# A mixture-of-experts layer: the second expert's weights are chosen and loaded before the last tokens are routed

## The reference, cut to what matters

```
logits = x @ w_gate                       # (2304, 8)
e_idx  = argmax(logits, axis=1)
gate_w = softmax(logits)[e_idx]
eom    = 1 / (1 + exp(-(x @ w_output_gate)))
for e in range(8):
    mask = e_idx == e
    if not mask.any(): continue
    h  = maximum(x[mask] @ w1[e], 0)      # 512 -> 1024
    ye = h @ w2[e]                        # 1024 -> 512
    out[mask] = gate_w[mask] * eom[mask, e] * ye
```

## Time and profile before

| | us |
|---|---|
| median of 3 runs (907.34 to 909.07) | 908.56 |
| the profiled execution | 907.39 |
| its span, first to last instruction | 905.5 |
| PE busy | 874.1 (97%) |
| DVE busy | 395.5 (44%) |
| ACT busy | 268.3 (30%) |
| POOL busy | 163.6 (18%) |
| DMA traffic | 68.50 MB, mean 76 GB/s |

### The profile page before, as it was taken

One profiled execution on the slowest core, in us unless ns is written; L12 is line 12 of the kernel. 1 busy time (PEld: TensorE's weight loads), 2 busy tenths in 40 slices (PEclk: granted clock), 3 DMA queues, 4 the chain that ended last, 5 costly groups with the idle time before them and its releaser, 6 DMA issues.

```text
span 905.5 us, 21892 instructions
## 1 busy us (share of the span) xinstructions
PE 874.1 (97%) x8248; PEld 784.0 (87%) x8249; DVE 395.5 (44%) x872; ACT 268.3 (30%) x499; POOL 163.6 (18%) x226
## 2 busy tenths in 40 slices
PE   8999999999999999999999999999979999999994
PEld 6888898989999898999989999898758888888883
DVE  5777885324233242333424233245754233624431
ACT  4564453222222122222212122226233113423311
POOL 5875301600000000000000000000123322323321
PEclk9999999999999999999999999999999999999997
DMA  9885733301010100001000010005161115216100
GB/s 264 245 233 165 234 113 114 95 12 36 4 44 0 39 8 12 35 0 46 0 23 23 12 35 0 24 1 210 34 224 47 35 46 183 85 38 213 52 25 19
DMA packets 52898, 68.50 MB, mean 76 GB/s; under 512 B 11886, under 2 KB 37614, under 8 KB 52848
## 3 DMA queue, kind: packets, MB, share of 16 engines
q1 hardware_dynamic: 46000, 45.20, 15.6%
q0 software_dynamic: 6560, 22.56, 8.1%
q10 hardware_dynamic: 288, 0.02, 0.0%
HBM read 54.11 MB, written 14.70 MB: 76 GB/s over the span
## 4 chain that ended last, share of the span: by engine, by line
PE 90%; DMA 3%; issue 2%; DVE 2%; SPq 1%; ACT 0%; POOLq 0%; POOL 0%; ACTq 0%; DVEq 0%
PE bank L1213 35%; PE bank L1234 15%; PE bank L1328 11%; PE bank L1356 11%; PE bank L1105 4%; PE bank L1182 4%; PE bank L1129 4%; PE bank L1343 2%; DMA e_w<-w 2%; PE bank L1165 1%; PE bank L1279 1%; PE bank L1243 1%; PE bank L1203 1%; DMA k_sb<-kT 1%; PE bank L1252 1%
## 5 line engine op out<-in xcount | busy, mean ns | idle before, releaser
L888 DVE TENSOR_TENSOR prod<-silu,bank 128x256 f32<-128x256 f32 x108 | 45.5, 421 | 209.5 <-ACT silu L597 209.2
L1213 PE MATMUL bank<-x_hi,wg_hi 128*128 128x256 f32 x432 | 125.2, 290 | 0.0
L1213 PE MATMUL bank<-x_hi,wv_hi 128*128 128x256 f32 x432 | 122.3, 283 | 0.0
L1213 PE MATMUL bank<-x_lo,wv_hi 128*128 128x256 f32 x432 | 122.3, 283 | 0.0
L1213 PE MATMUL bank<-x_hi,wv_lo 128*128 128x256 f32 x432 | 122.2, 283 | 0.0
L1213 PE MATMUL bank<-x_hi,wg_lo 128*128 128x256 f32 x432 | 122.1, 283 | 0.0
L1213 PE MATMUL bank<-x_lo,wg_hi 128*128 128x256 f32 x432 | 122.1, 283 | 0.0
L597 ACT ACTIVATE silu<-bank 128x256 f32<-128x256 f32 x108 | 41.5, 384 | 247.7 <-PE bank L1213 247.7
L1234 PE MATMUL bank<-wo_hi,h_hi 128*128 128x512 f32 x216 | 86.7, 401 | 0.0
L1234 PE MATMUL bank<-wo_hi,h_lo 128*128 128x512 f32 x216 | 84.5, 391 | 0.0
L1234 PE MATMUL bank<-wo_lo,h_hi 128*128 128x512 f32 x216 | 84.2, 390 | 0.0
(11 more groups left out here) (207 smaller groups left out, 1610.5 us busy)
## 6 DMA issues: line engine op xcount, KB each, us to landing
e_w<-w SPq DMA_DIRECT2D x32, 512.0 KB, 6.1
stage<-w_out POOLq DMA_DIRECT2D x16, 384.0 KB, 4.1
x_in<-x_rows SPq DMA_DIRECT2D x9, 512.0 KB, 3.6
y_rows<-y_sb SPq DMA_DIRECT2D x18, 256.0 KB, 2.0
k_sb<-kT SPq DMA_DIRECT2D x16, 256.0 KB, 5.1
v_sb<-v SPq DMA_DIRECT2D x16, 256.0 KB, 4.7
q_sb<-qT SPq DMA_DIRECT2D x16, 256.0 KB, 4.0
x_rows<-x_sb SPq DMA_DIRECT2D x16, 256.0 KB, 3.4
```

What stands on the lines that cost most here:

```text
L888: dve.tensor_tensor(prod[:, c % 2, :], silu[:, c % 2, :], bank[2 + c % 2][:, 0:GT], ALU.mult).then_inc(prod_ready, 1)
L1213: mm = pe.matmul(acc[:, 0:GT], w[:, k, cols], x[:, k, :], start=(k == 0 and i == 0), stop=(k == KC - 1 and i == 2))
```

## The change

VectorE also picks the expert with the second highest count of groups 0 to 7, behind chunk 8 of the last group, and puts it second in the order. SP loads it into the second half of `e_w` as soon as the last y rows are on their way and `y_done` is reached. It no longer waits for the table and the third gather, and the loop for rank 1 goes. As the choice is made before the last 256 rows are known, the second expert's count is raised to at least 1 (`second_c`), so that it has a tile whatever comes. In `load_chunk`, waits with known values use constants.

```diff
-        first_e = sb("first_e", [1, 1], I32)
+        first_e = sb("first_e", [1, 2], I32)
+        second = sb("second", [P, E])
+        second_c = sb("second_c", [P, E])
...
             def load_chunk(e, j, c):
-                if c >= HALF or not isinstance(j, int):
+                if not isinstance(j, int):
                     sp.wait_ge(e_raw[c % HALF], alone(sp, j * 32 + 16 * (c // HALF)))
+                elif j or c >= HALF:
+                    sp.wait_ge(e_raw[c % HALF], j * 32 + 16 * (c // HALF))
...
             store_y(NG - 1)
             sp.wait_ge(y_done, NG * TT)
+            sp.wait_ge(second_known, 1)
+            second_no = sp.value_load(first_e[0:1, 1:2], min_val=0, max_val=E - 1)
+            for c in range(CH):
+                load_chunk(second_no, 1, c)
...
             sp.wait_ge(tab_ready, 1)
             used = sp.value_load(table[0:1, T_USED:T_USED + 1], min_val=1, max_val=E)
-            sp.wait_ge(xg_in, 48)
-            with sp.If(used > 1):
-                with sp.Fori(1, 2) as j:
-                    load_expert(j)
...
-                dve.tensor_copy(first_e[:], keys[0:1, 3, 1:2]).then_inc(first_known, 1)
-                then(dve.tensor_scalar(keys[:, 1], rev[:], keys[:, 3, 0:1], -float(E), ALU.is_equal, ALU.mult))
-                then(dve.tensor_tensor(keys[:, 2], iota_f[:, 0:E], keys[:, 1], ALU.add))
+                dve.tensor_copy(first_e[0:1, 0:1], keys[0:1, 3, 1:2]).then_inc(first_known, 1)
+                then(dve.tensor_scalar(keys[:, 1], rev[:], keys[:, 3, 0:1], -2.0 * E, ALU.is_equal, ALU.mult))
+
+            def choose_second():
+                then(dve.scalar_tensor_tensor(out=second_c[:], in0=keys[:, 1], scalar=float(NT), in1=count[:],
+                                              op0=ALU.mult, op1=ALU.add))
+                then(dve.tensor_reduce(keys[:, 3, 3:4], second_c[:], AX.X, ALU.max))
+                then(dve.tensor_scalar(second_c[:], second_c[:], keys[:, 3, 3:4], None, ALU.is_ge))
+                then(dve.tensor_tensor(second_c[:], second_c[:], rev[:], ALU.mult))
+                then(dve.tensor_reduce(keys[:, 3, 4:5], second_c[:], AX.X, ALU.max))
+                then(dve.tensor_scalar(second[:], rev[:], keys[:, 3, 4:5], None, ALU.is_equal),
+                     dve.tensor_scalar(keys[:, 3, 5:6], keys[:, 3, 4:5], -1.0, float(E), ALU.mult, ALU.add),
+                     dve.tensor_tensor(keys[:, 2], iota_f[:, 0:E], keys[:, 1], ALU.add))
+                dve.tensor_copy(first_e[0:1, 1:2], keys[0:1, 3, 5:6]).then_inc(second_known, 1)
+                then(dve.scalar_tensor_tensor(out=keys[:, 2], in0=second[:], scalar=-float(E), in1=keys[:, 2],
+                                              op0=ALU.mult, op1=ALU.add))
                 then(dve.tensor_tensor(no_later[:], ...), dve.tensor_tensor(earlier[:], ...))
...
                         choose_first()
+                    if last and c == 8:
+                        choose_second()
...
             one_hots(NG - 1)
+            chained[0] = NG * STEPS_R + STEPS_0 + FIRST
+            then(dve.tensor_tensor(second_c[:], count[:], second[:], ALU.max))
             h_low(0, 1)
...
-            counts = count[:].rearrange("p (e o) -> p e o", o=1).to_broadcast([P, E, TILES])
+            counts = second_c[:].rearrange("p (e o) -> p e o", o=1).to_broadcast([P, E, TILES])
```

More of the change, by code:

```diff
@@ L229, in build @@
         early_ready = sem("early_ready")
+        second_known = sem("second_known")
         early_at_ready = sem("early_at_ready")
@@ L928, in _ @@
                 group(g, False, False)
-            FIRST = 14
+            FIRST = 22
             hidden(NG - 1, False, last=True)
@@ L975, in _ @@
             add_places(NG - 1)
-            chained[0] = NG * STEPS_R + STEPS_0 + FIRST
             dve.wait_ge(y_done, NG * TT)
```

## The result

The changed kernel takes 900.6 us (median of 4 runs, 900.13 to 901.35) against 908.35 for the kernel before (4 runs, 907.34 to 909.07): a ratio of 0.9916, interval 0.9899 to 0.9933. Its profiled execution took 900.67 us with a span of 899.0.

A forecast was written before the change was run, and what follows sets the result against it. TensorE held nine tenths of the chain, so only PE's idle or slow time could be won: -5.38 - 1.78 + 1.1 + 0.65 + 0.45 = -4.96 us, giving 903.6 us against the median of 908.56; range 901.9 to 905.8.

The forecast's parts named there:

- The stall and the clock: PE at tile 2: the 5.38 us wait for relu and 1.78 us of half-speed clock behind it are won.
- What stays on ScalarE: ScalarE's copies of the second expert still wait for the table, so 1.1 us of PE's relu wait stays.
- The new wait on VectorE: VectorE's share for the second expert delays h_low of tile 2, a new PE wait of 0.65 us.
- The gather beside the load: The second early gather lands in 7.2 us beside the load; PE waits 0.5 us, 0.45 together with VectorE's added level.
- VectorE's added level: One more level ahead of h_low(0, 1) on VectorE costs 0.2 us, overlapping the gather's delay.
- The risk: Rival: the early gather lands late behind the load, PE waits up to 10.1 us, 915.1 us in all; chance 0.05.

The follow-up runs named there:

- experiment 4: The changed kernel with the second expert's load put back behind the table and the third gather, new choice kept: 903.77 us, ratio 0.9961.
- experiment 3: The kernel before with only the second expert's load moved early, the expert's number written into the program: 903.4 us, ratio 0.9944.
- experiment 5: The kernel before, unaltered, run once more on another chip: 907.21 us, ratio 1.0003.
- experiment 6: The changed kernel, unaltered, run once more on another chip: 901.22 us, ratio 0.9928.
- experiment 1: The kernel before with 64 unused bytes added to tile credit, shifting the SBUF tiles behind it: 907.07 us, ratio 0.9993.
- experiment 2: The changed kernel with 64 bytes taken from tile credit, which undoes the SBUF shift: 900.64 us, ratio 0.9922.
- experiment 9: The kernel before with eleven idle memsets more on VectorE, behind the last group's chunk 8: 907.55 us, ratio 0.9996.
- experiment 10: The kernel before with one unused semaphore more: 906.42 us, ratio 0.999.
- experiment 8: The changed kernel with the second expert's weights copied one tile later on ScalarE and VectorE: 899.64 us, ratio 0.9913.
- experiment 7: The kernel before, load still late, with the second expert's weights copied one tile later on ScalarE and VectorE: 905.41 us, ratio 0.9976.

## Why the prediction was right in its mechanism and wrong in its number

**The stall and the clock** (-5.38 and -1.78): right. The wait of 5.4 us is replaced by the short ones, the clock holds at 1.00, and experiment 4 brings both back, the wait at 3.5 us, by putting the load alone in its old place.

**What stays on ScalarE** (+1.1): 0.98. The copies start at 663.96; the forecast's 665.1 less the 1.17 us by which the whole stretch is earlier is 663.93.

**The new wait on VectorE** (+0.65): 0.52, behind the stall and for `h_low(2, 0)`, as said.

**The gather beside the load** (with VectorE's added level, +0.45): the term of the stretch that was furthest off. PE didn't wait for the gather, so only the step of VectorE's queue, put at 0.2 us, can have remained. The forecast had the gather 0.4 us ahead of the load, took its place as of no account for the size of the term, and priced it by the first early gather, which is issued 0.7 us behind the load beside it. In the profile it was 1.6 us ahead and landed in 5.4 us, not in 7.2. The risk was real: level with the load, in experiment 3, PE waited 2.2 us for just this gather. In the five profiles that keep the changed kernel's early load the lead was 1.0 to 2.0 us, and GpSimd's moment varies by itself (17.3 to 18.8 us behind the first expert's first chunk over all profiles), so a part of this lead is luck.

By these terms the sum should have been -5.38 - 1.78 + 0.98 + 0.52 + 0.20 = -5.46, and the tail measures -5.33. Against -4.96 this is an error of 0.4 us, and inside the range. That it fits so well is in part two errors that cancel, as the starts on PE show (before, then after, beside the rows at 668.40 and 671.39 above):

```profile
668.08 0.39 PE L1328 MATMUL bank<-e_hi,xgT_lo 128*128 x1
673.85 1.12 PE L1343 MATMUL bank<-ident,h_sb 128*128 128x128 f32 x4 [5.38 <-ACT h_sb L662]
677.28 0.60 PE L1279 MATMUL bank<-ident,xg 128*128 128x128 f32 x4
677.63 0.48 PE L1356 MATMUL bank<-e_hi,hT_hi 128*128 x1
```

```profile
667.02 0.39 PE L1352 MATMUL bank<-e_hi,xgT_lo 128*128 x1
670.27 0.60 PE L1303 MATMUL bank<-ident,xg 128*128 128x128 f32 x4
```

From the last product to the turns of h are 5.77 us before and 1.38 after, -4.39, as -5.38 and +0.98 say. From there to the turns of rows are 3.43 and 1.87, so the clock gave 1.56 and not 1.78. From there to `layer2` are 0.35 and 1.12, so the wait for `h_low` cost 0.77 and not 0.52. Ahead of all this 0.11 is lost between the first chunk and the last product (51.19 and 51.30), where 0.20 was put. Together -5.07. The other 0.26 lies behind: 0.08 up to the turn of the last tile's rows, and 0.18 from there to the end.

**The rest is outside the stretch,** and there the forecast failed. Its step was "On the profiled execution: 907.39 - 4.96 = 902.4. That execution was 1.17 us under the median of 908.56; against the median the forecast is **903.6 us**", and it failed in two ways. It added 1.17 us because the profiled execution lay under the median of three runs. In the 65 later runs of the same kernel the medians are 907.1 to 907.3, and the profiled 907.39 was the better basis. And it had no term for anything before the first expert's load, without giving a reason, where the attention stage of the profiled execution was 1.40 us shorter. The measured 900.6 lies 3.0 us under the forecast: 1.17 are the basis, 0.37 the stretch, 1.40 less the 0.23 of the feed-forward stage are what stands ahead of it, and 0.3 is left between the spans and the medians. Either the basis or the stages ahead of the stretch, put right alone, would have left the lower end of the range at 900.7, still 0.1 above the measured; both together would have held it. The 7.75 us of the result are themselves on the high side, since its kernel before had a median of 908.35; the later sets give 5.9 to 6.6.

**Is the shorter attention stage the change's work?** Its variation is that of PE's issue waits, and a program that does the kernel before's work has shown 189.7 us once while its median didn't move. So single profiles can't settle it. The medians lean to yes: they differ by 5.9 to 6.6 us in the two later comparisons, where the tails differ by 5.0 (experiments 5 and 6) and 5.2 (1 and 2). All six profiles of changed programs have 192.53 us or less in this stage, and six of seven of the kernel before and its variants 193.31 or more. None of the differences tried alone (experiments 1, 3, 9, 10) shortens the stage beyond doubt. Whether the changed programs make long issue waits shorter by about 1 us, or the fifteen executions of experiments 2 and 6 and the result happened to fall well, stays open, and so does what PE waits for there. Late instruction fetches are a rival that wasn't tested: the traces have 29 packets on an instruction queue in the first 190 us, before and after alike.

## What to carry to other kernels

Where an in-order queue holds a needed instruction behind one that isn't due for seven tiles, either the data must come early or the instruction must move; here the first won 5.3 us of the 7.2 that the place could give, the second alone 1.4 (286.81 against 288.25), and both together 1.3 more than the first (experiments 8 and 6), in the tail. Issue a small transfer that is due soon ahead of a large one (here 1.0 to 2.0 us were enough), and look for every small lookup that would fall under the large one. Don't move the forecast to the median of three runs that spread as widely as the term in question. And cut the span into stages before comparing: a sum for one stretch can be right to 0.4 us while the total is off by three.

## What the runs showed of the chip that was not expected

- The latency of a 128-row gather beside a 4 MB load went with how far ahead of it it was issued: 2.0 us ahead, landed after 4.6 us (experiment 8), which is as without a load beside it; 1.6 ahead, 5.4 (the changed kernel); 1.2 ahead, 6.5 (experiment 6); level with it, 9.0 until PE ran (experiment 3). That is one execution each. The page "DMA: Bandwidth & Descriptors" of the Trainium skill, section "Queues, rings and completion order", has the DMA engines take turns between queues packet by packet, from which the prediction made an estimated 0.6 us more than alone. Against the 4.3 to 4.9 us alone, 5.4 agrees with that; 6.5 and 9.0 are more. Why, the rows don't show.
- A scale lookup of 128 values took 6.2 us to land in the midst of the load (experiment 7), against 2.4 and 3.0 without it (experiment 8 and the changed kernel). VectorE stood idle for 9.1 us up to the first of these, and for 5.4 in experiment 8.
- A shift of 64 bytes in SBUF cost 0.22 us in 423, in all five profiles that had it (423.17 to 423.19 against 422.96 or 422.97 in the eight others). Which tile does it wasn't looked for.
- PE's issue waits in the attention stage sum to 1.6 to 6.2 us from one execution to another. Their cause wasn't tested.
- At the same place the half clock lasted 3.4 us in the kernel before and 6.7 in experiment 1, after the same wait of 5.4 us, and read in half microseconds about 6.8 in experiments 5, 9 and 10, after 5.1 to 5.8. In the first the clock fell as the wait ended, in the others 2 to 3 us into it.
